# Two expert layers behind an attention: four passes by way of DRAM, three of them with seven half-size products

## What is computed

```python
# attention, for each of 8 x 8 heads: q, k, v are 576 x 64, phi is 576 x 32
a = exp(phi - max over tokens);  a = a / (sum over tokens + 1e-9)
k_m = a^T k;  v_m = a^T v                      # 32 x 64 each
attn = softmax(q k_m^T / 8)                    # 576 x 32
x = attn v_m                                   # 4608 tokens x 512
# layer 1
h = x @ w1_in                                  # 512 -> 2048
g = where(h > 0, h, exp(min(h, 0)) - 1)
y = g @ w1_out                                 # 2048 -> 512
# layer 2
h = y @ w2_in                                  # 512 -> 2048
g = h * clip(h + 3, 0, 6) / 6
out = g @ w2_out                               # 2048 -> 512
```

## Time and profile before

| | us |
|---|---|
| median of 3 runs | 1707.05 |
| lowest, highest | 1704.69, 1707.21 |
| the profiled execution: time of the run | 1707.1 |
| the profiled execution: span from the first to the last instruction | 1705.4 |
| TensorE busy in the span | 1607.6 (94%) |
| VectorE, ScalarE, GpSimd busy | 903.3, 596.7, 284.8 |

### The profile page before, as it was taken

One profiled execution on the slowest core, in us unless ns is written; L12 is line 12 of the kernel. 1 busy time (PEld: TensorE's weight loads), 2 busy tenths in 40 slices (PEclk: granted clock), 3 DMA queues, 4 the chain that ended last, 5 costly groups with the idle time before them and its releaser, 6 DMA issues.

```text
span 1705.4 us, 25865 instructions
## 1 busy us (share of the span) xinstructions
PE 1607.6 (94%) x9808; PEld 1413.9 (83%) x9808; DVE 903.3 (53%) x1595; ACT 596.7 (35%) x1187; POOL 284.8 (17%) x165
## 2 busy tenths in 40 slices
PE   4789999998999989999999999999999999999999
PEld 3688888887988879889998888888888888888887
DVE  3667667666676666766665434343434343433333
ACT  2544444343443443444344322222222222222222
POOL 2533113031040220402126201010101010100000
PEclk9899999999999999999999999999999999999999
DMA  9322212221222212220313010101000000101000
GB/s 237 107 63 50 56 36 50 63 46 36 51 60 50 56 35 53 50 63 15 138 39 113 0 50 1 50 0 45 5 28 21 18 31 3 46 0 49 0 25 25
DMA packets 178104, 79.52 MB, mean 47 GB/s; under 512 B 152400, under 2 KB 160592, under 8 KB 178000
## 3 DMA queue, kind: packets, MB, share of 16 engines
q1 hardware_dynamic: 168528, 76.07, 17.1%
q10 hardware_dynamic: 9472, 2.07, 0.8%
HBM read 59.24 MB, written 18.87 MB: 46 GB/s over the span
## 4 chain that ended last, share of the span: by engine, by line
PE 55%; issue 29%; POOL 7%; DVE 5%; ACT 3%; ACTq 1%; POOLq 0%; DVEq 0%
PE ps L291 18%; PE ps L293 18%; PE ps L292 18%; POOL ws_lo L750 6%; DVE g L671 2%; POOL rows L766 1%; DVE g L673 1%; ACT g L523 1%; ACT g_hi L525 1%; PE ps L312 0%; DVE g_lo L675 0%; ACTq L577 0%; ACT ws_hi L501 0%; PE ps L339 0%; ACT w_out_hi L511 0%
## 5 line engine op out<-in xcount | busy, mean ns | idle before, releaser
L291 PE MATMUL ps<-g_hi,w_out_lo 128*128 128x288 f32 x1024 | 314.7, 307 | 4.5 <-DVE g_lo L675 3.1
L292 PE MATMUL ps<-g_lo,w_out_hi 128*128 128x288 f32 x1024 | 302.5, 295 | 0.0
L293 PE MATMUL ps<-g_hi,w_out_hi 128*128 128x288 f32 x1024 | 302.3, 295 | 0.0
L681 DVE TENSOR_SCALAR g<-g 128x512 f32<-128x512 f32 x144 | 84.4, 586 | 370.4 <-ACT g L531 369.4
L671 DVE TENSOR_SCALAR g<-g 128x288 f32<-128x288 f32 x256 | 168.5, 658 | 142.1 <-ACT g L523 141.1
L525 ACT CAST g_hi<-g 128x288 fp32r<-128x288 f32 x256 | 110.8, 433 | 350.5 <-DVE g L673 350.5
L531 ACT ACTIVATE g<-ps,three 128x512 f32<-128x512 f32 x144 | 99.3, 690 | 376.6 <-PE ps L293 375.6
L291 PE MATMUL ps<-x_hi,w_in_lo 128*128 128x512 f32 x576 | 224.2, 389 | 0.0
L293 PE MATMUL ps<-x_hi,w_in_hi 128*128 128x512 f32 x576 | 224.1, 389 | 0.0
L292 PE MATMUL ps<-x_lo,w_in_hi 128*128 128x512 f32 x576 | 224.1, 389 | 0.0
L291 PE MATMUL ps<-w_out_hi,g_lo 128*128 128x512 f32 x576 | 224.1, 389 | 0.0
(11 more groups left out here) (126 smaller groups left out, 2437.2 us busy)
## 6 DMA issues: line engine op xcount, KB each, us to landing
layer_out<-y_sb SPq DMA_DIRECT2D x16, 576.0 KB, 3.1
x_raw<-layer_out SPq DMA_DIRECT2D x9, 1024.0 KB, 6.8
kv<-in_k SPq DMA_DIRECT2D x60, 144.0 KB, 3.5
kv<-in_v SPq DMA_DIRECT2D x60, 144.0 KB, 3.5
q<-in_q SPq DMA_DIRECT2D x60, 144.0 KB, 2.9
w_in_raw<-in_moe_w_in SPq DMA_DIRECT2D x8, 1024.0 KB, 11.2
w_out_raw<-in_moe_w_out SPq DMA_DIRECT2D x8, 1024.0 KB, 6.2
out<-out_sb SPq DMA_DIRECT2D x8, 1024.0 KB, 5.0
```

The lines of the kernel that those rows point to most:

```text
L291: nc.tensor.matmul(dst, a_lo, b_hi, start=first, stop=False)
L292: nc.tensor.matmul(dst, a_hi, b_lo, start=False, stop=False)
L293: return nc.tensor.matmul(dst, a_hi, b_hi, start=False, stop=last)
L681: nc.vector.tensor_scalar(g, g, 6.0, 1.0 / 6.0, ALU.min, ALU.mult).then_inc(e_clipped, 1)
```

## The change

The program is rewritten into four passes over all 4608 tokens.

Pass 1 (`batch`, eight of 576 tokens, 16 steps each) makes attention, the items and the first hidden layer, and stores it to DRAM (`hidden1`). A step is `up1` (twelve matmuls of 288 columns for both halves of the batch), on ScalarE `Relu` and `Exp`, and on VectorE one operation of 128x576. Two groups of attention go along the 16 steps of a batch, by a table of stages (`BATCH`). The sum over the tokens is now made on VectorE over the rows of a partition (`rows_sum`) and finished on TensorE with a column of ones. Beside this, GpSimd, ScalarE and SyncE make the forms of the weights for the later passes (seven sums or differences of quarters, each hi and lo) and store them in DRAM.

Passes 2 (`y_block`, y = g w1_out, 9 blocks), 3 (`up_block`, h and g of layer 2, 8 batches) and 4 (`down_block`, out = g w2_out, 9 blocks) split each matrix product in quarters and make seven half-size products in place of eight. Sums of the quarters of the tokens' side are made on VectorE, sums of the products on VectorE and ScalarE in PSUM and SBUF. In passes 2 and 4 a block has 14 grains of 24 matmuls of 256 columns, with a ring of three buffers for hi and lo; in pass 3 a step has 42 matmuls of 288 columns. Pass 3 stores the second hidden layer in DRAM (`hidden2`). The eight tiles of weight forms (1.8 MB each) are loaded anew for each of the three passes.

The table of stages, the new wait in `S_KV` and a batch on TensorE:

```diff
+        BATCH = {
+            0: ((S_Q0, EVEN), (S_PHI, ODD)), 1: ((S_Q1, EVEN), (S_MAX, ODD)), 2: ((S_KMT, EVEN),),
+            3: ((S_SC, EVEN), (S_SUB, ODD)), 4: ((S_BACK, EVEN), (S_KV, ODD)), 5: ((S_Q0, ODD), (S_EXP, EVEN)),
+            6: ((S_Q1, ODD), (S_KMT, ODD), (S_NORM, EVEN)), 8: ((S_PT, EVEN),),
+            9: ((S_SC, ODD), (S_PHI, NEXT)), 10: ((S_BACK, ODD), (S_MAX, NEXT)), 11: ((S_EXP, ODD),),
+            12: ((S_NORM, ODD), (S_SUB, NEXT)), 13: ((S_KV, NEXT),), 14: ((S_PT, ODD),)}
...
                 elif stage == S_KV:
                     pe.wait_ge(a_exp_made, g + 1)
...
+                            nc.tensor.matmul(t.ps_kv[rows], t.rows_a[0:ROWS, h, j], t.kv[0:ROWS, :, h, j],
+                                             start=(j == 0), stop=(j == CH - 1))
+                    pe.wait_ge(rows_sum_made, g + 1)
+                    nc.tensor.matmul(t.ps_a_sum, t.rows_sum[0:ROWS], one[0:ROWS], start=True, stop=True).then_inc(kv_done, 1)
...
+            def batch(b, par):
+                for f in range(FC):
+                    up1(b, f, par)
+                    for i, n, g in items_at(b, f):
+                        item(i, n, g, 4)
+                    for stage, g, n in stages_at(b, f):
+                        attention(g, stage, A, b > 0, n == ODD)
```

The hidden layer of pass 1 on ScalarE and VectorE:

```diff
-                nc.scalar.activation(g1[f % 2][:], hid(at, HALF), ACT.Exp).then_inc(e_made, 1)
-                nc.scalar.copy(g1_hi[:, f % RING], g1[f % 2][:]).then_inc(g_hi_made, 1)
+                nc.scalar.activation(e1[f % 2][:], ps[:, 2 * (f % 2):2 * (f % 2) + 2, 0:HALF], ACT.Relu, scale=-1.0).then_inc(r_made, 1)
+                nc.scalar.activation(e1[f % 2][:], e1[f % 2][:], ACT.Exp, scale=-1.0).then_inc(e_made, 1)
-                nc.vector.tensor_scalar(g, g, 1.0, -1.0, ALU.min, ALU.add).then_inc(e_clipped, 1)
-                nc.vector.tensor_tensor(g, g, hid(at, HALF), ALU.max).then_inc(turn_over, 1)
-                nc.vector.tensor_tensor(g_lo, g, g_hi.bitcast(F32), ALU.subtract).then_inc(g_lo_made, 1)
+                nc.vector.scalar_tensor_tensor(g1[f % 4][:], e1[f % 2][:], -1.0, ps[:, 2 * (f % 2):2 * (f % 2) + 2, 0:HALF],
+                                               ALU.add, ALU.max).then_inc(g_made, 1)
```

A grain of pass 2 on TensorE, with the order of products and halves (pass 4 is alike, with `DOWN = (1, 6, 5, 7, 2, 4, 3)`):

```diff
+        ORDER1 = ((1, 0), (5, 0), (6, 0), (1, 1), (6, 1), (5, 1), (7, 0), (7, 1), (2, 0), (3, 0), (4, 0), (2, 1), (3, 1), (4, 1))
...
+            def y_grain(i, q):
+                (k, h), slot = ORDER1[q], grain_slot(q)
+                pe.wait_ge(xg_ready, GRAINS * i + q + 1)
+                for j in range(FH // 2):
+                    for s in range(2):
+                        fj = h * (FH // 2) + j
+                        a = forms_of[fj][:, s]
+                        mm = three_passes(ps[:, BANK1[k] + s, 0:SUB], a[:, 0, LEFT[k]], a[:, 1, LEFT[k]],
+                                          ring_hi_1[slot][:, j], ring_lo_1[slot][:, j], k in (1, 6, 5) and fj == 0, fj == FH - 1,
+                                          onto=k in (7, 2, 4, 3))
+                mm.then_inc(xg_used, 1)
@@ pass 3, TensorE: order of the seven products in a step
+                    up_open(n, f, buf, f)
+                    if f > 0:
+                        up_close(n - 1, f - 1, buf, f - 1)
...
+                    up_middle(n, f, buf, f)
```

SyncE's tiles of forms between passes 2 and 3, and between 3 and 4:

```diff
+            sp.wait_ge(xg_used, GRAINS * last + 11)
+            load_tile(1, 0)
+            load_tile(1, 1)
+            store1(last)
+            load_tile(1, 2)
+            load_tile(1, 3)
+            sp.wait_ge(xg_used, GRAINS * BLOCKS)
+            for j in range(4, FH):
+                load_tile(1, j)
+            sp.wait_ge(stored, 16 * BLOCKS)
+            load_xc(1, 1)
+            for f in range(FH):
+                store_g(0, f)
...
+            for f in range(FH):
+                if f > 0:
+                    sp.wait_ge(up_done[3], STEPS2 - FH + f)
+                    load_tile(2, f - 1)
+                store_g(B - 1, f)
+            sp.wait_ge(up_done[3], STEPS2)
+            load_tile(2, FH - 1)
```

More of the change, by code:

```diff
@@ L77, in place @@
             return nc.alloc_sbuf_tensor_at(name, [P] + shape, dt, offset=base + offset)
+        tile = [place(f"tile{j}", [2, 2, 7, P], F32, t0 + j * TILE) for j in range(FH)]
+        forms_of = [a[:].bitcast(F32R) for a in tile]
         w_in_hi = place("w_in_hi", [DC, F], F32R, 0)
@@ new lines, in build @@
+        NS = 3 + 4 * CH * MAC
+        small = ctx.enter_context(nc.sbuf_tensor("stats", [P, NS + 2], F32))
+        small_b = ctx.enter_context(nc.sbuf_tensor("stats_b", [P, NS], F32))
+        one, one_half = small[:, NS:NS + 1], small[:, NS + 1:NS + 2]
+        KVQ = 109824
+        A = attention_set("", KVQ, 5, 6, small, row_max, rows_sum, kmT)
+        at = A.end
+        pT_at = (at, at, tail, tail)
+        pT_hi = [place(f"pT_hi{i}", [S], F32R, pT_at[i] + i % 2 * PT_BYTES) for i in range(4)]
@@ L107, in build @@
+        pT_lo = [place(f"pT_lo{i}", [S], F32R, pT_at[i] + i % 2 * PT_BYTES + S * 4) for i in range(4)]
+        at += 2 * PT_BYTES
         vT_hi = place("vT_hi", [2, 2, P], F32R, at)
@@ new lines, in build, with stage @@
+        B_ = attention_set("_b", at + 1536, 4, 2, small_b, row_max_b, rows_sum_b, kmT_b)
+        assert B_.end <= KVQ
+        def stage(tag, at):
+            return Stage(place("forms" + tag, [2, 7, P], F32, at),
+                         [sem(n + tag) for n in ("raw_loaded", "sum_made", "hi_made", "lo_made", "forms_stored")])
+        stage_a = [stage(f"_a{i}", t0 + i * PIECE) for i in range(2)]
+        stage_b = stage("_b", tail + 3 * SUB * 8 + DC * BLOCK * 4)
+        stage_c = stage("_c", 2 * W)
@@ L449, in _ @@
[L449 to L461 removed]
+            for b in range(B):
+                batch(b, b % 2)
@@ new lines, in _ @@
+            attention(2, S_PHI, A, 2)
+            for b in range(B):
+                batch(b, b % 2)
+            y_block(0, 0)
+            with dve.Fori(1, BLOCKS - 2, 2) as i:
+                y_block(i, 1)
+                y_block(i + 1, 0)
+            y_block(BLOCKS - 2, 1)
+            y_block(BLOCKS - 1, 0)
+            up_block(0, 0)
+            up_block(1, 1)
+            with dve.Fori(2, B - 3, 2) as u:
+                up_block(u, 0)
+                up_block(u + 1, 1)
+            up_block(B - 2, 0)
@@ L821, in _ @@
[L821 to L830 removed]
+            for n in range(6, NI):
+                split_in_lo(n)
+            for b in range(B - 1):
+                batch(b)
@@ new lines, in _ @@
+            load_phi(0)
+            load_kv(0)
+            load_in(0)
+            load_q(0)
+            for i in range(1, FB):
+                load_in(i)
+            sp.wait_ge(kv_done, 1)
+            load_phi(2)
+            load_kv(2)
+            follow_q(0, 2)
+            for b in range(B):
+                batch(b)
+            for n in range(4):
+                sp.wait_ge(g1_stored[n], 16 * STEPS1 // 4)
+            y_block(0)
+            with sp.Fori(1, BLOCKS - 1) as i:
+                y_block(i)
```

1659 lines of the change are left out of this document (1096 added, 563 removed).

## The result

| | us |
|---|---|
| before, median of 4 runs | 1706.28 |
| changed kernel, median of 4 runs (lowest, highest) | 1776.27 (1775.19, 1779.07) |
| ratio to before, 95% interval | 1.0414 (1.0396 to 1.0432) |
| span of the profiled execution | 1774.1 |

The account below looks back on a forecast made before the run. Streamed matmul columns on TensorE were taken as the bound. Opening and pass 1 506, pass 2 370, border 24, pass 3 371, border 20, pass 4 378, last store 5: span 1674, time 1676 us, range 1595 to 1755.

Parts of the forecast that it names:

- Columns: Matmuls of all passes: seven half-size products cut streamed column time from 1482.2 to 1369.2 us, a gain of 113 us.
- the line's value: Passes 2 and 4: the line through matmuls of 288 and 512 columns gives 119.3 ns for 256 columns.
- The rival that 256 cost what 288 do: Passes 2 and 4: a 256-column matmul costs 132.7 ns, adding 81 us, 1757 in all; chance 0.1.
- six weight loads 78 ns apart: Old trace: six loads of 128 weight columns about 78 ns apart, taken as support for the line at 256 columns.
- Pass 3's waits: Pass 3, step 2: `xc_sums` ahead of the sum product 7 needs costs 2 us a batch, 7 times; bounds 0 and 5.
- The clock: Pass 1: half clock after each gap at S_KV, 16 gaps x 3 = 48 us, 1722 in all; chance 0.06.
- A granted clock under 0.97: Profile after the change: a granted clock below 0.97 was named as a sign that the forecast is wrong.
- Pass 1: Pass 1: TensorE idles 3.6 us at step 4, about 4.4 + 3 at step 13; a batch 59.5 us, bounds 48 and 66.
- The opening: Start of the kernel: 43 us in place of 52, as ScalarE's 16 small loads become 7; bounds 38 and 55.
- The borders: Into and out of pass 3: queued tiles and stores cost 24 us and 20 us; bounds for the borders 15 and 75.
- DMA as a limit: Passes 2 to 4 and borders: stores and loads moving only 200 GB/s add 60 + 44 us, 1780; chance 0.17.
- the first rival: Pass 1 and borders: waits hide better, pass 1 at 50 us a batch, borders 20 us; 1590 us; chance 0.17.

Follow-up runs that it names:

- The three orders of pass 3: Changed kernel with, in pass 3, VectorE's sums one step later (1742.22 us), ScalarE's pieces at steps 3 and 7 (1734.47), or both, sums halved, loads issued earlier (1693.54).
- The fillers: Changed kernel plus unneeded matmuls in TensorE's waits: 40 of 224 columns per gap in pass 3 (1757.18 us); 28 with 64-column weights per group in pass 1 (1760.01).
- the sum moved: Changed kernel with VectorE's `rows_sum` at the head of its step in pass 1: 1727.29 us, ratio 1.0116 to the kernel before.
- a remedy for the second one: Changed kernel with down-form tiles issued before the stores out of pass 3, and tiles and quarters into pass 3 spread behind stores: 1766.7 us.
- a few such moves: Changed kernel with pass 3's, pass 1's and the borders' reorderings together, two copies moved forward and tile 4 behind the first store: 1611.5 us, ratio 0.944 to before.

## Why the prediction was wrong, step by step

- **Columns: right.** 119 ns for 256 columns was the line's value. Pass 2 was to take 370 us and took 370.0. The rival that 256 cost what 288 do is out. What the prediction took from six weight loads 78 ns apart, that loads don't bind at 256, came true by 7 ns: with 111.5 ns for 128 weight columns and the line's 12 ns and 0.42 a column, loads bind from some 240 columns down, by this estimate. The six loads were of transposes of plain f32 data; why theirs can be closer than those of fp32r products no run shows.
- **Pass 3's waits: the term that failed most.** It had 2 us a batch for `xc_sums` (bounds 0 and 5), from the sums' own length. The trace has two gaps, 9.7 us a batch. I had counted VectorE's work and not when its input lands: the load is issued one step ahead and needs 6.5 us, a step has 5.6. The second gap, ScalarE's wait for GpSimd's sums at step 5, had no term at all. The three orders of pass 3 show both: 34, 42 and 83 us.
- **The clock: it had 0.06 as a rival and nothing in the sum.** The prediction set it low since gaps of 1 to 2 us in the units left no trace. But the trace of before has one longer gap inside the stream, at the end of layer 1, behind the very operation of VectorE in the earlier trace rows that took 3.71 us:

```profile
901.21 0.61 PE L291 MATMUL ps<-g_hi,w_out_lo 128*128 128x288 f32 x1 [3.14 <-DVE g_lo L675]
...
901.86 0.44 PE L293 MATMUL ps<-g_hi,w_out_hi 128*128 128x288 f32 x1
902.10 0.44 PE L291 MATMUL ps<-g_hi,w_out_lo 128*128 128x288 f32 x1
```

  Matmuls of 288 columns come 0.24 us apart from there to 906.9, which costs 2.4 us. The sum itself forecast gaps of 3.6 and 4.4 us in pass 1, and the earlier trace rows showed half clock behind the opening's waits; all three were in hand, and the price should have stood in the sum and not beside it. A granted clock under 0.97 was named as a sign of being wrong, and it was 0.938. The fillers took back 21 us in pass 3 and 11 in pass 1. The rival's price, 3 us for each of 16 gaps, was too high for one gap and had too few of them.
- **Pass 1: the waits right in sum, the batch not.** At step 4 the wait for `rows_sum` was forecast as 3.6 us and was 4.6 to 5.0; at step 13 it was forecast as 4.4 behind 3 for the exponentials, and was 1.4 to 2.5 behind 2.3. A full batch (1 to 5) was to take 59.5 us and took 63.9 on average, of which 4.9 are slow time, which had no term. That the 59.0 left are near the forecast is in part luck: the errors of the waits cancel. With the sum moved a batch took 54.7 to 56.7. Batch 0 was to take 64 us and took 73.3, with 6.8 us of slow time. The opening took 49.7 us and not 43. TensorE's wait for the exponentials shrank from 10.3 to 7.3 us and `S_KV` began 4.2 us earlier; the number of loads was the wrong measure, since four of ScalarE's seven took 12.5 us to issue:

```profile
2.38 12.46 ACTq L940 DMA_DIRECT2D q_b<-in_q  x4
```

- **The borders: right.** Into pass 3 24 us were forecast and 22 waited (19.3 for u2 and 2.6 for a tile), by the stores behind the tiles, as said. Out of it 20 were forecast; waits of 1.7, 2.1, 2.9 and 11.3 us make 18. What was meant as a remedy for the second one did not work.
- **DMA as a limit: out.** With the waits gone pass 3 moved 231 GB/s instead of 181, and batches 1 to 6 have no gap over 1 us; what waits for transfers is at the borders.

In all the opening has 7 of the missing 100 us of span, pass 1 28, and passes 3 and 4 with their borders 65 (798 forecast, 863.5 taken). The design was not slower; its order was. The prediction had the columns and the wait that the code had added in the open; what decided were two waits a batch on loads, and the clock behind each. Some of the prediction's sums are off by 1 to 4 us (pass 2's 40.1 + 0.5 + 0.3 is 40.9 and not 41.1, the first rival's time 1586 and not 1590, the clock rival's 1724 and not 1722); none of it bears on the miss. That pass 2 came out as forecast, 370.0, is a little luck: the idle time was one gap of 4 us near its start, and not the late grains of each block. A block of pass 4 took 41.0 us and not 42: the 2 us at its end are not there.

## What to carry to other kernels

Where an engine waits in order for a transfer, set the issue's time and the transfer's own length against the step at which it is needed; the length of the instructions behind it says little. Price a gap of 3 to 5 us on TensorE with what the clock takes after it (0.8 to 2.4 us here), and look in the old trace for its one longest gap, which may show the price where the many short ones do not. When an order is changed, look at what now stands behind the moved transfer: at the second border the gain went into a new wait. When a rewrite with less work comes out slower, move single instructions by a step before giving it up: here a few such moves made 5.6% faster of 4.1% slower.
